# Token attention of a three-stage kernel: scores transposed, softmax in 32x32-block layout, part of it on Pool

## The reference

```
batch, n_heads, seq, head_dim = 8, 8, 576, 64 ; n_pack = 32
def sm_attn(qq, kk, vv):
    s = scale * np.matmul(qq, kk.transpose(0, 1, 3, 2))
    s = s - np.max(s, axis=-1, keepdims=True)
    a = np.exp(s)
    a = a / (np.sum(a, axis=-1, keepdims=True) + 1e-09)
    return np.matmul(a, vv)
p_packed = sm_attn(p, k, v)            # 32 pack rows per head
out = sm_attn(q, p_packed, p_packed)   # 576 tokens per head
```

## Time and profile before

| | us |
|---|---|
| median of 3 runs (1486.38 to 1493.37) | 1490.88 |
| profiled execution, its own time | 1501.39 |
| its span | 1499.6 |
| PE busy in the span | 1443.8 (96%) |
| DVE, ACT, POOL busy | 1009.9, 502.3, 524.8 |
| attention stage, from the start to the last sum of squares | 190.8 |

### The profile page before, as it was taken

How to read it: one execution, slowest core, us unless ns; L and a number is a source line. 1 busy time by engine, 2 the same in 40 slices (tenths; PEclk the granted TensorE clock), 3 DMA queues, 4 the chain that set the end, 5 groups by cost and what they waited for, 6 DMA issues and landing times. The chain is left out here.

```text
span 1499.6 us, 28719 instructions
## 1 busy us (share of the span) xinstructions
PE 1443.8 (96%) x10092; PEld 1314.0 (88%) x10093; DVE 1009.9 (67%) x1570; ACT 502.3 (33%) x796; POOL 524.8 (35%) x432
## 2 busy tenths in 40 slices
PE   8988889999999999999999999999999999999996
PEld 5767668878888888888899999999998999999996
DVE  4877764444444444444698888888898777777773
ACT  4765630033000102110554444444454333333331
POOL 0122267069760385250583333333260110011111
PEclk9999999999999999999999999999999999999998
DMA  8875276258751365233434444344475333334330
GB/s 319 308 283 221 104 259 135 82 183 265 177 188 42 115 211 178 98 123 112 162 113 141 127 126 121 117 131 123 147 250 194 118 139 126 122 129 140 140 113 29
DMA packets 141771, 232.77 MB, mean 155 GB/s; under 512 B 11528, under 2 KB 94856, under 8 KB 134160
## 3 DMA queue, kind: packets, MB, share of 16 engines
q1 hardware_dynamic: 104128, 145.50, 29.9%
q10 hardware_dynamic: 26448, 58.12, 11.7%
q0 software_dynamic: 11136, 28.40, 5.5%
HBM read 144.86 MB, written 87.12 MB: 155 GB/s over the span
## 5 line engine op out<-in xcount | busy, mean ns | idle before, releaser
L800 PE MATMUL ps<-wf,xf 128*128 128x256 f32 x3024 | 366.1, 285 | 4.4 <-DVE xf L1854 3.6
L800 PEld LDWEIGHTS ps<-wf,xf 128*128 128x128 f32 x3024 | 365.5, 193 | 5.0 <-DVE xf L1854 3.3
L800 PE MATMUL ps<-xf,wf 128*128 128x256 f32 x2646 | 323.8, 284 | 0.1
L800 PEld LDWEIGHTS ps<-xf,wf 128*128 128x128 f32 x2646 | 319.1, 192 | 0.3 <-ACT cb L1262 0.3
L800 PE MATMUL ps<-weights,xT 128*128 (+1 forms) x1032 | 247.5, 396 | 4.1 <-POOL weights L1996 2.9
L800 PE MATMUL ps<-weights,hT 128*128 (+1 forms) x1032 | 246.2, 394 | 0.8 <-DVE hT L1740 0.8
L800 PEld LDWEIGHTS ps<-weights,xT 128*128 128x128 f32 x1032 | 191.4, 189 | 44.2 <-issue 6.5
L800 PEld LDWEIGHTS ps<-weights,hT 128*128 128x128 f32 x1032 | 190.7, 188 | 39.2 <-issue 1.1
L1996 POOL TENSOR_TENSOR weights<-stage,weights 128x1024 fp32r<-128x1024 f32 x56 | 132.3, 2403 | 168.1 <-ACT weights L1131 168.1
L1131 ACT CAST weights<-stage 128x1024 fp32r<-128x1024 f32 x56 | 57.9, 1050 | 393.3 <-PE ps L800 296.4
L2105 POOL TENSOR_TENSOR h<-h,sg 128x512 f32<-128x512 f32 x72 | 100.8, 1400 | 187.0 <-ACT sg L1276 186.9
(11 more groups left out here) (222 smaller groups left out, 1855.9 us busy)
## 6 DMA issues: line engine op xcount, KB each, us to landing
g_rows<-h SPq DMA_DIRECT2D x144, 256.0 KB, 2.7
raw<-g_rows SPq DMA_DIRECT2D x36, 1024.0 KB, 4.9
stage<-w ACTq DMA_DIRECT2D x53, 512.0 KB, 3.7
w_forms<-fm ACTq DMA_DIRECT2D x16, 896.0 KB
x_in<-x_rows SPq DMA_DIRECT2D x43, 256.0 KB
y_rows<-y_sb SPq DMA_DIRECT2D x43, 256.0 KB
wf_f<-w_forms SPq DMA_DIRECT2D x11, 896.0 KB, 5.8
q_sb<-qT SPq DMA_DIRECT2D x8, 1152.0 KB
```

What stands on the lines that cost most here:

```text
L800: mm = pe.matmul(o, left(a_), right(b_), start=first and n == 0, stop=last and n == 2)
```

## The change

The token scores are made with the packs stationary: `scores_tokens(b, g)` makes, for a group of four heads, all 576 tokens' scores with the 4 x 32 packs on the partitions (banks 4 and 5, eight matmul records of 288 columns). DVE's block transpose turns each 32x32 block, so that a partition holds one token of each of 18 blocks, with 32 scores of one head in a row; `max_tokens` takes the 18 maxima. Pool subtracts them, ACT takes the exponential, DVE sums and inverts, Pool multiplies, and a second block transpose on DVE (`turn_weights`) gives the weights in the layout that `rows_tokens` wants, for all tiles at once. So PE's `turn_tokens` and ACT's `keep_aT` go, the softmax runs in two steps of 128x576 instead of five of 128x256, and `rows_tokens` of tile 0 waits for both groups. `keep_pl` moves from DVE to ACT. The order of all four `batch` functions is written anew, Pool's scatters of batch b-1 come behind its four softmax operations of batch b. In the last batch `rows_tokens` alternates between banks 6 and 7 and banks 4 and 5. `junk` moves into a stage slot.

```diff
-        tk_e = [a.put(f"tk_e{n}", [P, H, NPK], F32) for n in range(2)]
-        tk_a = [a.put(f"tk_a{n}", [P, H, NPK], F32) for n in range(2)]
-        tk_aT = [a.put(f"tk_aT{n}", [P, NG, P], F32) for n in range(2)]
+        tk_t = [a.put(f"tk_t{g}", [P, NBLK, NPK], F32) for g in range(NG)]
+        tk_aT = [a.put(f"tk_aT{g}", [P, S], F32) for g in range(NG)]
         x_row = [a.put(f"x_row{par}", [P, TPB, DM], F32) for par in range(2)]
...
-        junk = a.put("junk", [P, DM], F32)
+        last_slot = Shelf(nc, base, 16 * WLEN + NST * 4 * CH, 16 * WLEN + (NST - 1) * 4 * CH)
+        junk = last_slot.put("junk", [P, DM], F32)
...
-                sp.wait_ge(s2_done, TPB * (b - 2) + TPB)
+                sp.wait_ge(s2_done, 2 * (b - 2) + 2)
...
-            def scores_tokens(b, r, par, k, first):
+            def scores_tokens(b, r, par, g, first):
+                if g == 0:
+                    pe.wait_ge(q_in[par], 16 * (r + 1))
+                pe.wait_ge(ppt_kept, 2 * b + g + 1)
+                if not (first and g == 0):
+                    pe.wait_ge(t1_done, 2 * b + g)
+                for j in range(2):
+                    lo = 2 * NPK * j
+                    for n in range(2):
+                        mm = pe.matmul(bank[4 + n][lo:lo + 2 * NPK, 0:HALF], ppT[par][:, 2 * g + j, lo:lo + 2 * NPK],
+                                       q_sb[par][:, 2 * g + j, n * HALF:(n + 1) * HALF], start=True, stop=True)
+                mm.then_inc(s2_done, 1)
+            def rows_tokens(b, par, k, first, last=False):
...
+            def rows_tokens(b, par, k, first, last=False):
                 n, m = TPB * b + k, TOK[k]
                 if k == 0:
-                    pe.wait_ge(q_in[par], 16 * (r + 1))
-                    pe.wait_ge(ppt_kept, 2 * b + 2)
-                if not (first and k == 0):
-                    pe.wait_ge(sub_done, n)
-                for g in range(NG):
-                    for j in range(2):
-                        lo = 2 * NPK * j
-                        mm = pe.matmul(bank[4][0:m, g * P + lo:g * P + lo + 2 * NPK],
-                                       q_sb[par][:, 2 * g + j, k * P:k * P + m],
-                                       ppT[par][:, 2 * g + j, lo:lo + 2 * NPK], start=True, stop=True)
-                mm.then_inc(s2_done, 1)
-            def turn_tokens(b, par, k, first):
-                n = TPB * b + k
-                pe.wait_ge(a_done, n + 1)
-                if not (first and k == 0):
-                    pe.wait_ge(aT_kept, n)
-                a_t = tk_a[(par + k) % 2].rearrange("p h c -> p (h c)")
-                for g in range(NG):
-                    mm = pe.transpose(bank[5][:, g * P:(g + 1) * P], a_t[:, g * P:(g + 1) * P], ident)
-                mm.then_inc(aT_done, 1)
-            def rows_tokens(b, par, k, first):
-                n = TPB * b + k
-                pe.wait_ge(aT_kept, n + 1)
-                if k == 0:
+                    pe.wait_ge(aT_kept, 2 * b + 2)
                     pe.wait_ge(pl_kept, 2 * b + 2)
                 if not (first and k == 0):
-                    pe.wait_ge(x_kept, n)
-                    pe.wait_ge(lg_kept, n)
+                    behind = 1 if last and k else 0
+                    pe.wait_ge(x_kept, n - behind)
+                    pe.wait_ge(lg_kept, n - behind)
+                lo = row_bank(b, k)
                 for g in range(NG):
-                    mm = pe.matmul(bank[6 + g][:, 0:XW], tk_aT[(par + k) % 2][:, g, :], rhs[par][g],
+                    mm = pe.matmul(bank[lo + g][0:m, 0:XW], tk_aT[g][:, k * P:k * P + m], rhs[par][g],
                                    start=True, stop=True)
                 mm.then_inc(x_done, 1)
...
                 scores_tokens(b, r, par, 0, first)
                 if first:
-                    stay_warm(2, o=5)
-                if not first:
-                    turn_tokens(b - 1, other, 3, False)
-                logits_packs(b, par, 0)
-                if not first:
-                    if last:
-                        stay_warm(WARM)
-                    rows_tokens(b - 1, other, 2, False)
-                scores_tokens(b, r, par, 1, first)
-                if first:
-                    stay_warm(2, o=5)
+                    stay_warm(2, o=6)
                 if not last:
                     scores_packs(b + 1, rn, other, 1)
                 if not first:
-                    turn_tokens(b - 1, other, 4, False)
+                    rows_tokens(b - 1, other, 2, False)
+                scores_tokens(b, r, par, 1, first)
+                logits_packs(b, par, 0)
                 logits_packs(b, par, 1)
-                if last:
-                    stay_warm(WARM)
                 if not first:
                     rows_tokens(b - 1, other, 3, False)
-                scores_tokens(b, r, par, 2, first)
                 if first:
-                    stay_warm(2, o=5)
-                turn_tokens(b, par, 0, first)
+                    stay_warm(2, o=6)
                 if not last:
                     turn_packs(b + 1, 0)
                 if last:
                     stay_warm(WARM)
                 if not first:
                     rows_tokens(b - 1, other, 4, False)
-                scores_tokens(b, r, par, 3, first)
-                turn_tokens(b, par, 1, first)
+                if last:
+                    stay_warm(2 * WARM)
                 if not last:
                     values_packs(b + 1, rn, other, 0)
                     turn_packs(b + 1, 1)
-                if last:
-                    stay_warm(WARM)
-                rows_tokens(b, par, 0, first)
-                if not last:
                     turn_values(b + 1, other, 0)
-                scores_tokens(b, r, par, 4, first)
-                if not last:
-                    values_packs(b + 1, rn, other, 1)
-                    if more:
-                        scores_packs(b + 2, r + 1, par, 0)
-                turn_tokens(b, par, 2, first)
-                if not last:
-                    turn_values(b + 1, other, 1)
                 if not first:
                     pe.wait_ge(pl_kept, 2 * b + 2)
                     if not last:
                         pe.wait_ge(turn_kept, 2 * b + 4)
                     ranks(b - 1, other)
                 if last:
-                    stay_warm(WARM)
-                rows_tokens(b, par, 1, first)
+                    stay_warm(2 * WARM)
+                if not last:
+                    values_packs(b + 1, rn, other, 1)
+                rows_tokens(b, par, 0, first, last)
+                if not last:
+                    if more:
+                        scores_packs(b + 2, r + 1, par, 0)
+                    turn_values(b + 1, other, 1)
+                rows_tokens(b, par, 1, first, last)
...
+            def keep_pl(b, par, g):
+                act.wait_ge(pl_done, 2 * b + g + 1)
+                act.copy(rhs[par][g][:, 4 * D:XW], bank[2][:, 0:E]).then_inc(pl_kept, 1)
+            def exp_tokens(b, g):
+                act.wait_ge(sub_done, 2 * b + g + 1)
+                act.activation(tk_t[g], tk_t[g], ACT.Exp, scale=SCALE).then_inc(texp_done, 1)
...
-                x_ps = ps[0:m, 6:8, 0:4 * D]
+                x_ps = ps[0:m, row_bank(b, k):row_bank(b, k) + 2, 0:4 * D]
                 act.copy(x_row[par][0:m, k, :].rearrange("p (g c) -> p g c", g=NG), x_ps)
+                if isinstance(b, int) and b == B - 1:
+                    act.wait_ge(x_kept, n)
...
                     exp_packs(b + 1, 0, False)
-                exp_tokens(b, par, 0)
                 if not first:
-                    keep_aT(b - 1, other, 3, False)
                     keep_x(b - 1, rn, other, 2, False)
-                exp_tokens(b, par, 1)
-                first_hi(b, r, par)
                 if not last:
                     exp_packs(b + 1, 1, False)
+                exp_tokens(b, 0)
+                keep_pl(b, par, 0)
+                keep_pl(b, par, 1)
+                first_hi(b, r, par)
                 if not first:
-                    keep_aT(b - 1, other, 4, False)
                     keep_x(b - 1, rn, other, 3, False)
-                exp_tokens(b, par, 2)
-                keep_aT(b, par, 0, first)
                 if not last:
                     keep_turn(b + 1, 0, False)
+                exp_tokens(b, 1)
                 if not first:
                     keep_x(b - 1, rn, other, 4, False)
-                exp_tokens(b, par, 3)
-                keep_aT(b, par, 1, first)
                 if not last:
                     keep_turn(b + 1, 1, False)
-                if not last:
                     keep_ppt(b + 1, other, 0, first)
                 keep_x(b, r, par, 0, fresh)
-                exp_tokens(b, par, 4)
-                keep_aT(b, par, 2, first)
                 if not last:
                     keep_ppt(b + 1, other, 1, first)
...
+            def max_tokens(b, g):
+                G = 2 * b + g
+                dve.wait_ge(s2_done, G + 1)
```

(87 more changed lines are left out.)

52 lines of the change are left out of this document (12 added, 40 removed).

## The result

The kernel after takes 1524.8 us (median of 4 runs, 1524.0 to 1531.3), the kernel before beside it 1492.1 (4 runs): a ratio of 1.0236, 95% interval 1.0195 to 1.0276, or +32.7 us. The forecast was 1511, +20.5. The profiled execution of after took 1524.0, its span is 1522.2.

A forecast was written before the change was run, and what follows sets the result against it. No engine is full; the order of the queues in the attention stage sets the period. Six periods +22.8, last period +2, first rows +2 and the end -6.4 gave +20.5: 1511 us, likeliest case 1503 to 1518, range 1497 to 1522.

The forecast's parts named there:

- step 4: From tile 3's copy through tile 4, expert choice, group 1's sum, diagonal and second transpose, queued in VectorE's order: 9.9 us.
- The base: Period of one attention batch in the kernel before, without VectorE's idle times by "remote": 18.9 us.
- holds: VectorE idle by "remote" before the second tile's max, during Pool's scatters, in the kernel before: some 12 us over six batches.
- First rows: Start of the attention stage: first rows come some 2 us later, behind a softmax of two groups of 576.
- Last period: Last attention period, without its pack half: 19.8 us against 17.8 in the old chain, +2.
- The end: From tile 0's rows in the last batch to the last sum of squares: 7.9 us instead of 14.3, -6.4.
- Six periods: Tile 0 of batch 0 to tile 0 of batch 6: +3.8 us each, +22.8 in all.
- half clock in each batch: Rival, chance 0.10: TensorE at 1.2 GHz behind an idle stretch in each batch, +5 us (1516), at most +10 (1521).
- one sign of the forecast: In the profile after, PE is idle before turn_values and before the rows of tile 0.
- holds real and gone: Rival, chance 0.12: VectorE's "remote" idle times occur in all runs and vanish after the change, leaving 8.5 us: 1499.
- Transpose dear: Rival, chance 0.08: a block transpose of 128x576 costs 1.5 us, twice the price taken; +9 in seven periods: 1520.
- Totals decide: Rival, chance 0.10: engine work totals, not queue order, set the period; at 16.5 us, -17 in all: 1474.

The follow-up runs named there:

- e9: Kernel after with extra unused TensorE products filling its waits (27, 10, 10 and 9 at four places): 1516.4 us, ratio 1.0075 to the kernel before.
- e8: Kernel before with VectorE's loop over batches 3 and 4 written out: 1494.1 us, ratio 0.9998 to the kernel before.
- e5: Kernel after, unchanged, measured again: 1524.5 us, ratio 1.0202 to the kernel before.
- e10: Kernel after, unchanged, measured a third time: 1528.1 us, ratio 1.0144 to the kernel before.
- e4: Kernel before, unchanged, profiled once more: one execution of 1510.9 us, beside 1511.8 for the kernel before.
- e11: Kernel before, unchanged, profiled a third time: one execution of 1507.3 us, beside 1503.5 for the kernel before.
- e6: Kernel after, same operations, with the orders of TensorE, ScalarE and VectorE within a batch laid out anew: 1477.6 us, ratio 0.9881 to the kernel before.
- e16: Kernel after with those three queues reordered, plus extra unused TensorE products (9 a batch, 24 in the first): 1485.0 us, ratio 0.9849 to the kernel before.
- e14: Kernel after with extra unused TensorE products and tile 2's rows ahead of group 1's pack scores: 1516.1 us, ratio 1.0050 to the kernel before.
- e15: Kernel after with extra unused TensorE products, group 1's sum and group 0's diagonal ahead of tile 4's logits on VectorE: 1515.4 us, ratio 1.0041 to before.

## Why the prediction was wrong

**Right: the direction, and the chain at full clock.** The forecast's steps, put from copy to copy (the 1.17 us from rows to copy moved into step 4), against e9's four distances averaged over six periods and after's:

| step | forecast | e9, full clock | after |
|---|---|---|---|
| 1, tile 0 to 1 | 2.71 | 2.69 | 2.89 |
| 2, tile 1 to 2 | 4.46 | 4.57 | 4.58 |
| 3, tile 2 to 3 | 4.48 | 4.58 | 4.81 |
| 4, tile 3 to the next tile 0 | 11.07 | 11.17 | 12.59 |
| sum | 22.7 | 23.0 | 24.9 |

The base, 18.9 us without holds, is 18.80 in e8. First rows: +2 forecast, 35.3 against 33.6 us in e5 and e8, +1.7. Last period: +2, measured +2.3 (19.8 against 17.5). The end: -6.4; tile 0's copy of the last batch to the last copy takes 6.55 instead of 12.01, -5.5. Six periods: +22.8, measured 149.1 - 112.8 = +36.3. The four sum to +34.8, and the spans of e5 and e8 differ by 34.6 (the medians beside each other by 30.5: e8's profiled execution, 1487.7, was at the fast end of its own).

**Wrong: "half clock in each batch", put at nothing in the sum and too small as a rival.** It stood apart from the likeliest case, as a rival of chance 0.10 at +5, at most +10, worked out from one stretch of 3.4 us in a batch. The trace of after has 6.2 us a batch. The stretch behind the diagonal's wait is there in every batch, and twice it lasts 6.8 us (from 104.9 and from 156.0); three more, from about 122, 145.9 and 173.3, stand behind the 1.27 us wait of the second `logits_packs`, which the forecast does not name. Each us at 1.2 GHz costs 0.30 us of period (24.87 - 23.02 over 37 / 6), close to the quarter that the forecast took (half of a loss of one half), so 6 x 1.85 = 11.1 us; e9 beside e10 gives 11.7. With one stretch a batch it would have been 6. Of the 1.85 us a period 1.42 are in step 4. There the forecast lists TensorE with 0.7 for `turn_values` and `ranks` and leaves out `values_packs` of group 1, which stands between them and tile 0's rows: at full clock its 1.31 us are hidden beside the second transpose, at 1.2 GHz its 2.40 are not. So one sign of the forecast failed: in after, TensorE isn't idle ahead of the rows of tile 0 in any of the six batches. The rest is 6 x 0.3 of the chain, +1.8 (the parts were read a tenth short each), +0.9 of the end and +0.6 of the base. (In the traces the terms miss by 14.3 us, the medians by 12.2; e8's profiled execution was a fast one.) The mechanism was named and its price a us was right; the time at 1.2 GHz was not, and a thing that the one case in the trace and the rule both spoke for had been given 0.10 and no place in the sum. The Trainium skill's rule ("TensorE: Matmul & The Clock Gate", Why this matters for your kernels), that idle gaps between bursts bring the half clock back, agrees with the trace: the 2.89 us wait has 0.50 behind it, and filling it keeps 1.00.

**The base of the sum.** Taking the holds "for a matter of the profiled execution" gave the right sum beside medians of 1492 to 1494, and that was luck in part: e4, near the median of its measurement, has them too, so they are no matter of a profiled execution as such. The kernel before took 1492.1, 1511.8, 1494.0, 1503.5 and 1507.5 us in five measurements, the kernel after 1524.8, 1524.5 and 1528.1 in three. The rival "holds real and gone" may thus be partly true where they occur: beside 1503.5 the loss is 24.6 us, not 32.7, and no profile of after had any "remote". The 14 us at 1.2 GHz of e11 are in that smaller loss too, about 4 us at the price above.

**The other rivals.** Transpose dear: no, 0.775 us. Totals decide: no for this order, since undoing one piece of the queue took 13 us off; yes as a measure of what the order costs: the forecast put that case at periods of 16.5 and 1474 us, and e6 has 16.7 to 17.7 in five of six and 1477.6.

## What to carry to other kernels

Count all new waits of TensorE, not only the longest, price each stretch at half clock by its share on the chain, and put it into the sum: here it was a third of the loss. When a stretch can run at half clock, also list what TensorE does beside the chain, since at 1.2 GHz it may end last. This change, which makes five short softmaxes into two long ones, took the slack out of every queue; its gain in work (PE, DVE) showed only when the orders were laid out anew, 47 us, of which 12 are the clock's. Matmuls that keep the clock are worth having while the wait lasts that they fill; when the wait goes, they are the path. Measure the kernel before more than once: its own medians differed by 20 us, three fifths of the effect.

## What the hardware showed unexpectedly

The kernel before, with TensorE busy for 87% of a period, had 3.4, 27 and 14 us at 1.2 GHz in three profiles, and its twin without the loop none and 14: the same program gets its full clock in one measurement and not in another, and which of chip and chance it is no run tells. In e4 the granted clock is 0.50 from about 59.0 us on for 13.7 us, though TensorE's longest waits in the ten us ahead were 0.70 and 0.47; e8 has waits of 0.69 and 0.48 at the same place and stays at 1.00. VectorE's holds by "remote", up to 3.7 us each, appeared in the attention stage in four of the five profiles of the kernel before and its twin, and in e16, while e14 and e15 had one each on ScalarE (1.8 and 2.5 us) and the three profiles of after none; no run explains them. A block transpose of 128x576 costs 0.77 us, as much as a reduction over the same elements (0.75), out of a bank and out of memory alike (775 and 766 ns).
